# Expert 0 in two tiles of 128 rows by halves of the tokens, one of them multiplied behind the dense layers

## The chip, the cores and the metric

The kernel runs on one core of a Trainium2 chip (trn2). Time is device time in microseconds; several runs are given with their median. TensorE (PE) multiplies, VectorE (DVE) and ScalarE (ACT) work on its results, GpSimd (POOL) works in SBUF and issues the indirect DMAs, SyncE (SP) issues the other DMAs.

## The reference

Three stages, one after the other, on 1536 tokens (2 sequences of 768) of 384 features:

```python
# 1: linear attention with decay, 8 heads of 48
y[t] = r[t] @ (state + (u*k[t]) outer v[t]);  state = w*state + k[t] outer v[t]
# 2: dense layers, 384 -> 2048 -> 384
h = x @ w_in;  x2 = elu(h) @ w_out
# 3: mixture of 8 experts, one per token, capacity 384 rows each
e = argmax(x2 @ w_gate);  gate = softmax(x2 @ w_gate)[e]
out = gate * (relu(x2 @ w1[e]) @ w2[e])      # 384 -> 1024 -> 384
```

For these inputs 196 tokens choose expert 0: 96 in the first 768 tokens and 100 in the others. The fullest expert has 229.

## The kernel before, in words

Every matrix product of the dense layers and the experts is made of three fp32r products of parts (`product`, L1032): hi x hi, hi x lo, lo x hi. ScalarE makes the hi part of a weight or activation, VectorE or GpSimd the lo part.

*Dense loop.* `for n in range(NB)`: 6 blocks of 256 tokens, in each `for f in range(FT)`: 16 chunks of the 2048 features. Chunk f is 9 products of 256 columns (`fc1`, L1135) and, three chunks later, 6 products of 384 columns (`fc2`, L1149). In between go VectorE `min` (L920), ScalarE exp (L656), VectorE (L923), ScalarE g_hi (L658), GpSimd g_lo (L538). The attention of later chunks, the routing of the block before, and in block 5 the splitting of expert 0's weights (`expert0_hi` L646 for even f, `expert0_lo` L909 for odd f from 5) are placed by hand at fixed f. All engines run their lists in order; the order is written out in the code.

*Routing* of block n: `x2_rows`, `x2_transpose`, `x2_transposed`, `logits` (12 fp32 instructions of 8 columns), `shift`, `choose`, `count`, `gates`, `place_rows`, then `scatter_rows` (two indirect DMAs on GpSimd's queue) that put each token's row into the DRAM tensor `slots` at its expert's place. For blocks 0 to 4 this runs inside the next block; for block 5 nothing is left to run beside it.

*Between.* After the routing of block 5 TensorE makes `keep_busy(WARM_C)` = 9 fp32 products of 384 columns that nobody reads, waits for the scatters, makes `keep_busy(WARM_D)` = 4 more, and waits for expert 0's 256 rows. An fp32 product shows as two instructions.

*Experts.* `expert(i, r, more)` (L1264) does expert 2i+r on all engines: `expert_x` transposes its 256 rows, 8 chunks f of 9 products with 256 columns and 6 with 384. Weights of even experts lie in `we_*`, of odd ones in `wd_*`. SP loads the next weights when `fc1` (`s_he`) and `fc2` (`s_fc2e`) of the expert before last are done; at f=2 to 4 ScalarE makes the hi part of the next expert's W1 (L694), VectorE one f later the lo part (L984), at f=5 to 7 ScalarE W2 (L702), GpSimd its lo part (`split_w2`, L548). Experts with over 256 rows are finished in an overflow path that runs only if `n_over` is above 256.

## Time and profile before

| what | us |
|---|---|
| median of 3 runs | 455.81 (454.64 to 456.68) |
| profiled execution | 456.96 |
| its span | 455.2 |
| TensorE busy | 434.9 (96%) |
| VectorE busy | 243.1 (53%) |
| ScalarE busy | 183.1 (40%) |
| GpSimd busy | 235.0 (52%) |

The dense loop's last product starts at 288.2 us, expert 0's first at 307.4, expert 1's first at 325.4. Busy times of TensorE are modelled from pipelined instructions: a product's duration (0.28 us at 256 columns) is longer than the distance to the next one, so the pitch, the distance between two starts, is what a product costs. L1034, L1035 and L1036 are the three products of the helper `product`, wherever it is called from.

### The profile page before, as it was taken

The numbers are of one execution on the slowest core, as the hardware profiler recorded it, in microseconds if no ns is written. First come the engines' busy times: TensorE is split into PE (matmuls) and PEld (weight loads), VectorE is DVE, ScalarE is ACT, GpSimd is POOL, SyncE is SP. The second block draws the span as 40 slices with busy tenths as digits, with TensorE's granted clock in tenths as the row PEclk, the third lists the DMA queues.
The fourth block names the chain that finished last, engine by engine and source line by source line (L and its number), as shares of the span: only waits on it lengthen the run. The fifth ranks groups of instructions, "written<-read, shape, count | busy, mean of one in ns | idle before, by whom it ended". The sixth has DMA issues, their size and how long they took to land.

```text
span 455.2 us, 9620 instructions
## 1 busy us (share of the span) xinstructions
PE 434.9 (96%) x3796; PEld 412.9 (91%) x3796; DVE 243.1 (53%) x583; ACT 183.1 (40%) x392; POOL 235.0 (52%) x241
## 2 busy tenths in 40 slices
PE   8789999999999999999999999699999999999994
PEld 8679999999998999899999998559999999999994
DVE  7877864564465446644554575405454454553521
ACT  4255543233333333323233445104564464555520
POOL 1886785457656764675453325110725626527431
PEclk9989999999999999999999999889999999999999
DMA  7994874204111302020016002630548448357100
GB/s 255 380 403 142 291 248 177 104 8 136 37 73 25 120 16 94 18 79 2 1 29 286 0 1 56 257 104 1 208 142 329 159 186 330 114 221 291 51 30 26
DMA packets 16442, 61.80 MB, mean 136 GB/s; under 512 B 2050, under 2 KB 9118, under 8 KB 14352
## 3 DMA queue, kind: packets, MB, share of 16 engines
q1 hardware_dynamic: 14608, 56.49, 34.3%
q0 software_dynamic: 1792, 4.73, 2.8%
q8 instruction: 29, 0.48, 0.4%
q14 instruction: 13, 0.11, 0.1%
HBM read 49.38 MB, written 12.62 MB: 136 GB/s over the span
## 4 chain that ended last, share of the span: by engine, by line
PE 83%; DVE 6%; ACT 4%; DMA 2%; POOL 2%; issue 2%; SPq 0%; POOLq 0%; DVEq 0%
PE bank L1034 23%; PE bank L1036 21%; PE bank L1035 21%; PE bank L1228 2%; PE bank L1050 2%; PE bank L1075 2%; PE bank L1183 2%; ACT elu L656 1%; DMA rkt<-rkt 1%; DVE elu L923 1%; PE bank L1114 1%; PE bank L1244 1%; PE bank L1170 1%; PE bank L1110 1%; DVE we_lo L912 1%
## 5 line engine op out<-in xcount | busy, mean ns | idle before, releaser
L538 POOL TENSOR_TENSOR g_lo<-elu,g_hi 128x256 fp32r<-128x256 f32 x96 | 77.5, 807 | 106.6 <-ACT g_hi L658 106.2
L656 ACT ACTIVATE elu<-elu 128x256 f32<-128x256 f32 x96 | 40.2, 418 | 113.9 <-DVE elu L920 112.5
L1034 PE MATMUL bank<-xt,wd_hi 128*128 128x256 f32 x288 | 81.9, 284 | 1.2 <-DVE elu L923 1.2
L1035 PE MATMUL bank<-xt,wd_hi 128*128 128x256 f32 x288 | 81.4, 283 | 0.0
L1036 PE MATMUL bank<-xt,wd_lo 128*128 128x256 f32 x288 | 81.4, 283 | 0.0
L920 DVE TENSOR_SCALAR elu<-bank 128x256 f32<-128x256 f32 x96 | 40.4, 421 | 59.0 <-PE bank L1036 58.9
L1034 PE MATMUL bank<-wd_hi,g_hi 128*128 128x384 f32 x192 | 68.8, 358 | 1.5 <-POOL g_lo L538 1.5
L923 DVE SCALAR_TENSOR_TENSOR elu<-elu,bank 128x256 f32<-128x256 f32 x96 | 40.4, 421 | 49.7 <-ACT elu L656 49.7
L1035 PE MATMUL bank<-wd_lo,g_hi 128*128 128x384 f32 x192 | 64.9, 338 | 0.0
L1036 PE MATMUL bank<-wd_hi,g_lo 128*128 128x384 f32 x192 | 64.8, 337 | 0.0
L658 ACT CAST g_hi<-elu 128x256 fp32r<-128x256 f32 x96 | 39.0, 406 | 46.8 <-DVE elu L923 46.8
L977 DVE SCALAR_TENSOR_TENSOR ge_lo<-bank,ge_hi 128x256 fp32r<-128x256 f32 x64 | 27.2, 425 | 56.4 <-ACT ge_hi L689 56.4
L1034 PEld LDWEIGHTS bank<-xt,wd_hi 128*128 128x128 f32 x288 | 54.5, 189 | 2.7 <-DVE elu L923 2.3
L1036 PEld LDWEIGHTS bank<-xt,wd_lo 128*128 128x128 f32 x288 | 54.9, 191 | 0.0
L1035 PEld LDWEIGHTS bank<-xt,wd_hi 128*128 128x128 f32 x288 | 54.7, 190 | 0.0
L553 POOL TENSOR_TENSOR wd_lo<-wd_raw,wd_hi 128x1024 fp32r<-128x1024 f32 x12 | 28.5, 2403 | 46.7 <-ACT wd_hi L702 46.7
L689 ACT ACTIVATE ge_hi<-bank 128x256 fp32r<-128x256 f32 x64 | 24.7, 385 | 59.8 <-PE bank L1036 30.8
L1034 PEld LDWEIGHTS bank<-wd_hi,g_hi 128*128 128x128 f32 x192 | 36.5, 190 | 5.0 <-POOL g_lo L538 2.5
L1035 PEld LDWEIGHTS bank<-wd_lo,g_hi 128*128 128x128 f32 x192 | 36.5, 190 | 0.0
L1036 PEld LDWEIGHTS bank<-wd_hi,g_lo 128*128 128x128 f32 x192 | 36.3, 189 | 0.0
L553 POOL TENSOR_TENSOR we_lo<-we_raw,we_hi 128x1024 fp32r<-128x1024 f32 x9 | 21.4, 2402 | 24.5 <-ACT we_hi L702 24.5
L561 POOL DMA_INDIRECT out<-yrow,tok_i x16 | 15.7, 982 | 16.7 <-DVE yrow L997 13.2
(162 smaller groups left out, 978.3 us busy)
## 6 DMA issues: line engine op xcount, KB each, us to landing
we_raw<-wexp SPq DMA_DIRECT2D x8, 1536.0 KB, 7.1
wd_raw<-wexp SPq DMA_DIRECT2D x8, 1536.0 KB, 6.8
nat<-nat SPq DMA_DIRECT2D x10, 672.0 KB, 4.9
rkt<-rkt SPq DMA_DIRECT2D x12, 512.0 KB, 6.7
slots<-blank SPq DMA_DIRECT2D x2, 2316.0 KB, 11.9
xrow<-slots SPq DMA_DIRECT2D x16, 193.0 KB, 7.0
wd_raw<-win SPq DMA_DIRECT2D x4, 768.0 KB, 8.3
wd_raw<-wout SPq DMA_DIRECT2D x4, 768.0 KB, 10.4
```

What stands on the lines that cost most here:

```text
L538: nc.gpsimd.tensor_tensor(g_lo[:, f % 4, :], elu[:, f % 2, :], g_hi[:, f % 4, :].bitcast(F32), ALU.subtract).then_inc(s_glo, 1)
L553: nc.gpsimd.tensor_tensor(EL[r][:, cols], ER[r][:, cols], EH[r][:, cols].bitcast(F32), ALU.subtract).then_inc(s_elo2[r], 1)
L561: nc.gpsimd.indirect_dma_start(out=out, out_offset=bass.IndirectOffsetOnAxis(ap=tok_i[r][:, t, :], axis=0), in_=yrow[r][:, t, :], in_offse ...
L656: nc.scalar.activation(elu[:, f % 2, :], elu[:, f % 2, :], ACT.Exp).then_inc(s_exp, 1)
L658: nc.scalar.copy(g_hi[:, f % 4, :], elu[:, f % 2, :]).then_inc(s_ghi, 1)
L689: nc.scalar.activation(ge_hi[:, f % 4, :], ps_e[f % 2][:, 0:SN], ACT.Relu).then_inc(s_gehi, 1)
L920: V.tensor_scalar_min(elu[:, f % 2, :], ps_h[f % 2][:, 0:BN], 0.0).then_inc(s_m, 1)
L923: V.scalar_tensor_tensor(out=elu[:, f % 2, :], in0=elu[:, f % 2, :], scalar=-1.0, in1=ps_h[f % 2][:, 0:BN], op0=ALU.add, op1=ALU.max).then ...
L977: V.scalar_tensor_tensor(out=ge_lo[:, f % 4, :], in0=ps_e[f % 2][:, 0:SN], scalar=0.0, in1=ge_hi[:, f % 4, :].bitcast(F32), op0=ALU.max, o ...
L1034: mm(dst, w_hi, x_hi, start=start, stop=False)
L1035: mm(dst, w_hi, x_lo, start=False, stop=False)
L1036: return mm(dst, w_lo, x_hi, start=False, stop=stop)
```

## The change

Expert 0's rows are held in two tiles. Tokens of the first 768 (blocks 0 to 2, `EB` = 3) get slots 0 on, tokens of the others get slots from `LATE` = 3072 on; for that `slot0[:, 0:1]` is rewritten after block 2 from a total count (`ps_tot`), which `count` now makes for blocks 2 and 5 in front of the positions. `slots` has 27 tiles of 128 rows in place of 24.

SP loads the first tile behind expert 0's weights; TensorE transposes it at f=9 of block 5 (`early_x`), ScalarE and VectorE split it there. Behind the dense layers TensorE multiplies it (`early_fc1`, `early_fc2`: 8 chunks of 9 products with 128 columns and 3 with 384), in pieces between the routing steps of block 5 and after them. `WARM_C` goes from 9 to 2. The hi parts of expert 1's weights are made by ScalarE at early f=5 to 7 (W1) and late f=0 to 2 (W2), the lo part of W1 by VectorE in one go before the late tile. Then the second tile is loaded and multiplied in the same way as the first (late), with `expert_x` of expert 1 in it. The output rows of expert 0 are gated and scattered tile by tile. The total count for `n_over` is read on VectorE in six steps behind the early tile's gating; `n_over` is raised above 256 as well if either tile would hold over 128 rows, and the overflow path has three more turns. The diff, cut to its core:

```diff
...
-    NSB = NE * CAP // 128 // (NBLANK // 2)
+    EB = NB // 2
+    NOVER = NE + 3
+    LATE = NE * CAP
+    NSLOT = LATE + CAP
+    NSB = -(-NSLOT // 128 // (NBLANK // 2))
...
+        ps_tot = ps_y[1][:, C + 2 * BT * NE:C + 2 * BT * NE + NE]
...
-        WARM_A, WARM_B, WARM_C, WARM_D = 16, 8, 9, 4
+        WARM_A, WARM_B, WARM_C, WARM_D = 16, 8, 2, 4
...
+        F_A = 9
...
             sp.wait_ge(s_y, NSTEP)
             load_w(0, 0)
             load_w2(0, 0)
+
+            def load_part(t, row):
+                sp.dma_start(xrow[0][:, t, :], slots[row:row + 128, :]).then_inc(s_xr[0], 16)
+
+            for b in range(2):
+                sp.wait_ge(s_scat[b], 16 * BT * ((EB + 1 - b) // 2))
+            load_part(0, 0)
             sp.wait_ge(s_h, FT * NB)
             load_w(1, 1)
             load_w2(1, 1)
             for b in range(2):
                 sp.wait_ge(s_scat[b], 8 * NSTEP)
-            load_x(0, 0)
+            load_part(1, LATE)
             load_x(1, 1)
...
+                    scatter_tile(r, t)
+
+            split_w2(0, 1)
+            pool.wait_ge(s_atok, 1)
+            pool.wait_ge(s_ye[0], 1)
+            scatter_tile(0, 0)
+            pool.wait_ge(s_tok[0], 1)
+            pool.wait_ge(s_ye[0], 2)
+            scatter_tile(0, 1)
+            split_w2(1, 0)
+            scatter_out(0, 1)
+            with pool.Fori(1, NE // 2 - 1) as i:
                 split_w2(i, 1)
                 scatter_out(i, 0)
                 split_w2(i + 1, 0)
...
+                    if n == NB - 1 and f == F_A:
+                        act.wait_ge(s_axtr, 1)
+                        nc.scalar.copy(xe_hi[0][:, :, 0:C],
+                                       ps_s[0][:, 0:DM].rearrange("p (k n) -> p k n", k=KT)).then_inc(s_axhi, 1)
+
+            def early_hi(f):
+                act.wait_ge(s_ah, f + 1)
+                nc.scalar.activation(ge_hi[:, f % 4, 0:C], ps_e[f % 2][:, 0:C], ACT.Relu).then_inc(s_aghi, 1)
+
             x2_rows(NB - 1)
+            early_hi(0)
             x2_transposed(NB - 1)
+            early_hi(1)
             probs(NB - 1)
+
+
+            def expert1_hi(c):
+                act.wait_ge(s_w1[1] if c < N1 else s_w2[1], 16)
+                cols = slice(c * ECH, (c + 1) * ECH)
+                nc.scalar.copy(EH[1][:, cols], ER[1][:, cols]).then_inc(s_ehi[1], 1)
+
+            for f in range(2, ET):
+                early_hi(f)
+                if f >= ET - N1:
+                    expert1_hi(f - (ET - N1))
 
             def expert_x(i, r):
 
@@ -701,8 +764,16 @@
                         cols = slice(W1 + c * ECH, W1 + (c + 1) * ECH)
                         nc.scalar.copy(EH[nr][:, cols], ER[nr][:, cols]).then_inc(s_ehi[nr], 1)
 
-            expert_x(0, 0)
-            expert(0, 0, True)
+            act.wait_ge(s_xtr[0], 1)
+            nc.scalar.copy(xe_hi[0][:, :, C:SN],
+                           ps_xt[0][:, 0:DM].rearrange("p (k n) -> p k n", k=KT)).then_inc(s_xehi[0], 2)
+            for f in range(ET):
+                act.wait_ge(s_he, f + 1)
+                nc.scalar.activation(ge_hi[:, f % 4, 0:C], ps_e[f % 2][:, 0:C], ACT.Relu).then_inc(s_gehi, 1)
+                if f < N1:
+                    expert1_hi(N1 + f)
+                if f == F_X:
+                    expert_x(0, 1)
             expert(0, 1, True)
...
                 V.tensor_copy(slot_i[n % 2][:, :], there).then_inc(s_row, 1)
+                if n == EB - 1:
+                    link(V.tensor_copy(early0[:, :], ps_tot[:, 0:1]))
+                    link(V.tensor_scalar(slot0[:, 0:1], early0[:, :], -1.0, float(LATE), ALU.mult, ALU.add))
...
+                    if n == NB - 1 and f == F_A:
+                        dve.wait_ge(s_axhi, 1)
+                        V.tensor_tensor(xe_lo[0][:, :, 0:C], ps_s[0][:, 0:DM].rearrange("p (k n) -> p k n", k=KT),
+                                        xe_hi[0][:, :, 0:C].bitcast(F32), ALU.subtract).then_inc(s_axlo, 1)
+
+            def early_lo(f):
+                dve.wait_ge(s_aghi, f + 1)
+                V.scalar_tensor_tensor(out=ge_lo[:, f % 4, 0:C], in0=ps_e[f % 2][:, 0:C], scalar=0.0,
+                                       in1=ge_hi[:, f % 4, 0:C].bitcast(F32), op0=ALU.max,
+                                       op1=ALU.subtract).then_inc(s_aglo, 1)
+
+            def tokens_of(t, s):
+                dve.wait_ge(s_xr[0], 16 * (t + 1))
+                V.tensor_copy(tok_i[0][:, t, :], xrow[0][:, t, TOKEN:XR]).then_inc(s, 1)
+
+            def gated(t, y):
+                V.tensor_scalar(yrow[0][:, t, :], y, xrow[0][:, t, GATE:GATE + 1], None, ALU.mult).then_inc(s_ye[0], 1)
+
             x2_rows(NB - 1)
+            early_lo(0)
             x2_transposed(NB - 1)
+            early_lo(1)
             shift(NB - 1)
             choose(NB - 1)
+            early_lo(2)
             gates(NB - 1)
             place_rows(NB - 1)
-            dve.wait_ge(s_tot, 1)
-            V.tensor_reduce(col3[:, 1, 0:1], ps_y[0][:, 0:NE], AXX, ALU.max).then_inc(s_tables, 1)
-            dve.wait_ge(s_tables, NTAB + 1)
+            for f in range(3, ET):
+                early_lo(f)
+            tokens_of(0, s_atok)
+            dve.wait_ge(s_y0, 1)
+            gated(0, ps_y[0][:, 0:DM])
+            link(V.tensor_copy(part3[:, 0, :], ps_tot))
+            link(V.tensor_tensor(part3[:, 1, 0:1], part3[:, 0, 0:1], early0[:, :], ALU.subtract))
+            link(V.tensor_tensor(part3[:, 1, 1:2], part3[:, 1, 0:1], early0[:, :], ALU.max))
+            link(V.tensor_scalar_add(part3[:, 0, 0:1], part3[:, 1, 1:2], float(SN - C)))
+            link(V.tensor_reduce(col3[:, 1, 0:1], part3[:, 0, :], AXX, ALU.max))
             V.tensor_copy(n_over[:, :], col3[:, 1, 0:1]).then_inc(s_over, 1)
 
             def expert_x(i, r):
@@ -997,8 +1099,24 @@
                     V.tensor_scalar(yrow[r][:, t, :], ps_ye[t][:, 0:DM], xrow[r][:, t, GATE:GATE + 1], None,
                                     ALU.mult).then_inc(s_ye[r], 1)
 
-            expert_x(0, 0)
-            expert(0, 0, True)
+            for c in range(N1):
+                dve.wait_ge(s_ehi[1], c + 1)
+                cols = slice(c * ECH, (c + 1) * ECH)
+                V.tensor_tensor(EL[1][:, cols], ER[1][:, cols], EH[1][:, cols].bitcast(F32),
+                                ALU.subtract).then_inc(s_elo1[1], 1)
+            dve.wait_ge(s_xehi[0], 2)
+            V.tensor_tensor(xe_lo[0][:, :, C:SN], ps_xt[0][:, 0:DM].rearrange("p (k n) -> p k n", k=KT),
+                            xe_hi[0][:, :, C:SN].bitcast(F32), ALU.subtract).then_inc(s_xelo[0], 2)
+            for f in range(ET):
+                dve.wait_ge(s_gehi, f + 1)
+                V.scalar_tensor_tensor(out=ge_lo[:, f % 4, 0:C], in0=ps_e[f % 2][:, 0:C], scalar=0.0,
+                                       in1=ge_hi[:, f % 4, 0:C].bitcast(F32), op0=ALU.max,
+                                       op1=ALU.subtract).then_inc(s_gelo, 1)
+                if f == F_X:
+                    expert_x(0, 1)
+            tokens_of(1, s_tok[0])
+            dve.wait_ge(s_fc2e, ET)
+            gated(1, ps_ye[1][:, 0:DM])
...
+            def early_x():
+                pe.wait_ge(s_xr[0], 16)
+                for kt in range(KT):
+                    last = nc.tensor.transpose(ps_s[0][:, 128 * kt:128 * kt + 128],
+                                               xrow[0][:, 0, 128 * kt:128 * kt + 128], ident[:, :])
+                last.then_inc(s_axtr, 1)
+
             def x2_transpose(n, t):
                 pe.wait_ge(s_x2[t], n + 1)
                 pe.wait_ge(s_att, 2 * min(2 * n + 5, NSTEP))
+                if n == NB - 1:
+                    pe.wait_ge(s_axlo, 1)
...
                 pe.wait_ge(s_oh, n + 1)
+                if n in (EB - 1, NB - 1):
+                    pe.wait_ge(s_seen, n + 1)
+                    mm(ps_tot, ones[:, :], n_seen[:, :], start=True, stop=True)
                 mm(ps_cnt, earlier[:, :], onehot[:, :, :], start=True, stop=False)
                 mm(ps_cnt, ones[:, :], before[:, :, :], start=False, stop=True).then_inc(s_pos, 1)
...
+                    if n == NB - 1 and f == F_A:
+                        early_x()
...
+            def early_fc1(f):
+                wait_if(pe, s_aglo, f - 1)
+                if f == 0:
+                    pe.wait_ge(s_elo1[0], 2 * N1)
+                    pe.wait_ge(s_g, FT * NB)
+                for kt in range(KT):
+                    cols = slice(kt * FE + f * 128, kt * FE + (f + 1) * 128)
+                    last = product(ps_e[f % 2][:, 0:C], we_hi[:, cols], we_lo[:, cols], xe_hi[0][:, kt, 0:C],
+                                   xe_lo[0][:, kt, 0:C], kt == 0, kt == KT - 1)
+                last.then_inc(s_ah, 1)
+
+            def early_fc2(f):
+                pe.wait_ge(s_aglo, f + 1)
+                cols = slice(W1 + f * DM, W1 + (f + 1) * DM)
+                last = product(ps_y[0][:, 0:DM], ge_hi[:, f % 4, 0:C], ge_lo[:, f % 4, 0:C], we_hi[:, cols],
+                               we_lo[:, cols], f == 0, f == ET - 1)
+                if f == ET - 1:
+                    last.then_inc(s_y0, 1)
+
             for f in range(FT - LAG, FT):
                 fc2(NB - 1, f)
+            early_fc1(0)
             for t in range(BT):
                 x2_transpose(NB - 1, t)
+            early_fc1(1)
             logits(NB - 1)
+            early_fc1(2)
+            early_fc2(0)
             count(NB - 1)
-
-            pe.wait_ge(s_seen, NB)
-            mm(ps_y[0][:, 0:NE], ones[:, :], n_seen[:, :], start=True, stop=True).then_inc(s_tot, 1)
+            for f in range(3, ET):
+                early_fc1(f)
+                early_fc2(f - 2)
+            early_fc2(ET - 2)
+            early_fc2(ET - 1)
...
-            expert_x(0, 0)
-            expert(0, 0, True)
+            def late_fc2(f):
+                pe.wait_ge(s_gelo, f + 1)
+                cols = slice(W1 + f * DM, W1 + (f + 1) * DM)
+                last = product(ps_ye[1][:, 0:DM], ge_hi[:, f % 4, 0:C], ge_lo[:, f % 4, 0:C], we_hi[:, cols],
+                               we_lo[:, cols], f == 0, f == ET - 1)
+                last.then_inc(s_fc2e, 1)
+
+            pe.wait_ge(s_xr[0], 32)
+            for kt in range(KT):
+                last = nc.tensor.transpose(ps_xt[0][:, 128 * kt:128 * kt + 128], xrow[0][:, 1, 128 * kt:128 * kt + 128],
+                                           ident[:, :])
+            last.then_inc(s_xtr[0], 1)
+            pe.wait_ge(s_aglo, ET)
+            pe.wait_ge(s_xelo[0], 2)
+            for f in range(ET):
+                wait_if(pe, s_gelo, f - 1)
+                for kt in range(KT):
+                    cols = slice(kt * FE + f * 128, kt * FE + (f + 1) * 128)
+                    last = product(ps_e[f % 2][:, 0:C], we_hi[:, cols], we_lo[:, cols], xe_hi[0][:, kt, C:SN],
+                                   xe_lo[0][:, kt, C:SN], kt == 0, kt == KT - 1)
+                last.then_inc(s_he, 1)
+                if f >= 2:
+                    late_fc2(f - 2)
+                if f == F_X:
+                    expert_x(0, 1)
+            late_fc2(ET - 2)
+            late_fc2(ET - 1)
             expert(0, 1, True)
...
-            [np.concatenate([tiled(moe2_w1[e]), tiled(moe2_w2[e])], axis=1) for e in range(NE)])),
+            [np.concatenate([tiled(moe2_w1[e]), tiled(moe2_w2[e])], axis=1) for e in list(range(NE)) + [0]])),
```

## Rows read from the trace of the kernel before

**Rows 1.** Page, part 1: busy us of each engine, share of span, instructions

```profile
PE 434.9 (96%) x3796; PEld 412.9 (91%) x3796; DVE 243.1 (53%) x583; ACT 183.1 (40%) x392; POOL 235.0 (52%) x241
```

**Rows 2.** Chain of work that ended last, 262:288: start us, us, what

```profile
271.77 1.22 DVE we_lo L912
...
285.97 1.21 POOL g_lo L538
287.22 0.44 PE bank L1034
```

**Rows 3.** Timeline, 288:303: start us, us, engine, line, operation, xcount [idle before]

```profile
288.58 0.56 DVE L903 COPY x2row<-bank 128x384 f32<-128x384 f32 x1 [1.99 <-PE bank L1036]
...
289.11 0.87 PE L1170 MATMUL bank<-ident,x2row 128*128 128x128 f32 x6 [0.57 <-ACT x2row L636]
...
290.72 1.48 PE L1183 MATMUL bank<-gate_w,x2t 128*128 128x8 f32 x12 [0.74 <-DVE x2t L907]
292.31 0.17 DVE L864 TENSOR_REDUCE col<-bank 128x2 f32<-128x16 f32 x1 [1.65 <-PE bank L1183]
...
293.57 0.61 PE L1190 MATMUL bank<-onehot,earlier 128*128 128x16 f32 x2 [1.37 <-DVE before L873]
...
295.59 0.17 DVE L898 CAST slot_i<-prob 128x2 uint32<-128x2 f32 x1
...
301.44 1.75 SPq L388 DMA_DIRECT2D xrow<-slots  x4
```

**Rows 4.** Chain of work that ended last, 280:330, the idling products

```profile
295.02 10.96 PE bank L1228 x26
```

**Rows 5.** Source view of L388, 300:307: the first four row loads

```profile
DMA to landing us min/median/max: 2.5/2.9/3.7
```

**Rows 6.** Timeline, 306:311.5: first product of expert 0 and three later ones

```profile
307.41 0.36 PE L1278 MATMUL bank<-xe_hi,we_hi 128*128 128x256 f32 x1 [0.77 <-ACT xe_hi L681]
...
310.97 0.28 PE L1036 MATMUL bank<-xe_hi,we_lo 128*128 128x256 f32 x1
...
311.09 0.34 PE L1034 MATMUL bank<-we_hi,ge_hi 128*128 128x384 f32 x1
...
311.27 0.34 PE L1035 MATMUL bank<-we_lo,ge_hi 128*128 128x384 f32 x1
```

**Rows 7.** Timeline, 322:330: weight load, first product of expert 1, first use

```profile
322.66 0.35 SPq L381 DMA_DIRECT2D we_raw<-wexp  x1
...
325.44 0.28 PE L1278 MATMUL bank<-xe_hi,wd_hi 128*128 128x256 f32 x1
...
329.24 1.04 ACT L694 CAST we_hi<-we_raw 128x1024 fp32r<-128x1024 f32 x1
```

**Rows 8.** Groups by line and form, weight loads: xcount, busy us, mean ns

```profile
L1035 PEld LDWEIGHTS bank<-xe_lo,we_hi 128*128 128x128 f32 x84 | 15.8, 188 | 0.0
...
L1075 PEld LDWEIGHTS bank<-nat 128*64 128x64 f32 x320 | 10.2, 138 | 3.4 <-POOL nat L467 1.6 <-issue 0.9
L1183 PEld LDWEIGHTS bank<-gate_w,x2t 128*128 128x128 f32 x72 | 8.5, 191 | 1.6 <-issue 1.5
```

**Rows 9.** Groups by line and form, VectorE

```profile
L984 DVE TENSOR_TENSOR wd_lo<-wd_raw,wd_hi 128x1024 fp32r<-128x1024 f32 x12 | 14.6, 1216 | 0.0
...
L814 DVE TENSOR_TENSOR xt<-bank,xt 128x128 fp32r<-128x128 f32 x12 | 3.4, 281 | 0.0
...
L907 DVE COPY x2t<-bank 128x384 f32<-128x384 f32 x6 | 3.3, 552 | 0.9 <-PE bank L1170 0.9
```

**Rows 10.** Groups by line and form, ScalarE

```profile
L640 ACT COPY x2t<-bank 128x384 f32<-128x384 f32 x6 | 2.8, 473 | 0.6 <-PE bank L1170 0.6
```

**Rows 11.** Timeline, 28:31.5, TensorE

```profile
28.42 1.12 PE L1075 MATMUL bank<-nat 128*64 128x32 f32 x32 [1.36 <-POOL nat L467]
```

**Rows 12.** Windows: stretch, us, TensorE busy, granted clock, DMA share, GB/s

```profile
30.00:33.40 3.40, 3.40 (x16) 0.53 1.02 413
...
294.00:300.00 6.00, 6.00 (x13) 0.51 0.18 66
```

More of the change, by code:

```diff
@@ L89, in build @@
     col3 = new("col3", [128, 2, BT])
+    early0 = new("early0", [128, 1])
     slot_i = [new(f"slot_i{b}", [128, BT], U32) for b in range(2)]
@@ L108, in build, with expert_rows @@
     end_d = top[0]
+    def expert_rows(r):
+        return (new(f"xrow{r}", [128, 2, XR]), new(f"xe_hi{r}", [128, KT, SN], F32R),
+                new(f"xe_lo{r}", [128, KT, SN], F32R), new(f"yrow{r}", [128, 2, DM]),
+                new(f"tok_i{r}", [128, 2, 1], U32))
+    rows0 = expert_rows(0)
+    end_d = top[0]
     top[0] = x_at
-    xrow = [new(f"xrow{r}", [128, 2, XR]) for r in range(2)]
-    xe_hi = [new(f"xe_hi{r}", [128, KT, SN], F32R) for r in range(2)]
-    xe_lo = [new(f"xe_lo{r}", [128, KT, SN], F32R) for r in range(2)]
     ge_hi = new("ge_hi", [128, 4, SN], F32R)
     ge_lo = new("ge_lo", [128, 4, SN], F32R)
-    yrow = [new(f"yrow{r}", [128, 2, DM]) for r in range(2)]
-    tok_i = [new(f"tok_i{r}", [128, 2, 1], U32) for r in range(2)]
+    xrow, xe_hi, xe_lo, yrow, tok_i = zip(rows0, expert_rows(1))
     assert max(top[0], end_d) <= nc.sbuf_usable_end, (top[0], end_d)
@@ L238, in build @@
         s_sout = pair("out_scattered")
+        s_axtr = sem("early_x_transposed")
+        s_axhi = sem("early_x_hi_ready")
+        s_axlo = sem("early_x_lo_ready")
+        s_ah = sem("early_h_done")
+        s_aghi = sem("early_g_hi_ready")
+        s_aglo = sem("early_g_lo_ready")
+        s_atok = sem("early_tok_ready")
         s_dld = sem("d_loaded")
@@ L414, in _, with load_over @@
             with sp.If(over > SN):
-                def load_over(e):
+                def load_over(e, row):
                     sp.dma_start(we_raw[:, :], wexp[bass.ds(e, 1), :, :]).then_inc(s_dld, 16)
-                    sp.dma_start(xrow[0][:, 0, :], slots[bass.ds(e * CAP + SN, 128), :]).then_inc(s_dld, 16)
-                load_over(0)
-                with sp.Fori(1, NE) as e:
+                    sp.dma_start(xrow[0][:, 0, :], slots[bass.ds(row, 128), :]).then_inc(s_dld, 16)
+                load_over(0, SN)
+                with sp.Fori(1, NE + 1) as e:
                     sp.wait_ge(s_dout, 16 * e)
-                    load_over(e)
-                sp.wait_ge(s_dout, 16 * NE)
+                    load_over(e, e * CAP + SN)
+                with sp.Fori(0, 2) as j:
+                    sp.wait_ge(s_dout, 16 * (j + NE + 1))
+                    load_over(j * NE, j * LATE + C)
+                sp.wait_ge(s_dout, 16 * NOVER)
         @block.gpsimd
@@ L516, in scatter_rows @@
                 pool.wait_ge(s_row, n + 1)
-                pool.reg_add(last_slot, one, NE * CAP - 2)
+                pool.reg_add(last_slot, one, NSLOT - 2)
                 nc.gpsimd.indirect_dma_start(
@@ L554, in split_w2, with scatter_tile @@
                                             ALU.subtract).then_inc(s_elo2[r], 1)
+            def scatter_tile(r, t):
+                pool.reg_add(last_token, one, T - 2)
+                nc.gpsimd.indirect_dma_start(
+                    out=out, out_offset=bass.IndirectOffsetOnAxis(ap=tok_i[r][:, t, :], axis=0),
+                    in_=yrow[r][:, t, :], in_offset=None, bounds_check=last_token,
+                    oob_is_err=False).then_inc(s_sout[r], 16)
             def scatter_out(i, r):
@@ L559, in scatter_out @@
                     pool.wait_ge(s_ye[r], 2 * i + t + 1)
-                    pool.reg_add(last_token, one, T - 2)
-                    nc.gpsimd.indirect_dma_start(
-                        out=out, out_offset=bass.IndirectOffsetOnAxis(ap=tok_i[r][:, t, :], axis=0),
-                        in_=yrow[r][:, t, :], in_offset=None, bounds_check=last_token,
-                        oob_is_err=False).then_inc(s_sout[r], 16)
-            with pool.Fori(0, NE // 2 - 1) as i:
+                    scatter_tile(r, t)
[9 more added lines that the diff above has]
+            with pool.Fori(1, NE // 2 - 1) as i:
                 split_w2(i, 1)
@@ L576, in _ @@
             with pool.If(over > SN):
-                with pool.Fori(0, NE) as e:
+                with pool.Fori(0, NOVER) as e:
                     pool.wait_ge(s_dye, e + 1)
@@ L714, in _ @@
             with act.If(over > SN):
-                with act.Fori(0, NE) as e:
+                with act.Fori(0, NOVER) as e:
                     act.wait_ge(s_dld, 32 * (e + 1))
@@ L1010, in _ @@
             with dve.If(over > SN):
-                with dve.Fori(0, NE) as e:
+                with dve.Fori(0, NOVER) as e:
                     dve.wait_ge(s_dhi, e + 1)
@@ L1305, in _ @@
             with pe.If(over > SN):
-                with pe.Fori(0, NE) as e:
+                with pe.Fori(0, NOVER) as e:
                     pe.wait_ge(s_dld, 32 * (e + 1))
```

11 lines of the change are left out of this document (6 added, 5 removed).

## The prediction

> **What bounds the kernel now.** I read the page's busy shares first: TensorE is busy 434.9 of 455.2 us [rows 1], so what can still be won lies where it works on nothing useful. The chain of work that ended last says where that is. It runs on TensorE through nearly the whole span; the exceptions are the last dense block and the stretch behind it. In the second half of the last dense block the chain goes through VectorE: at f=9 the placing of rows and a 1.22 us split of expert 0's weights hold back the next `elu` step, and the chain stays on VectorE, ScalarE and GpSimd until 287.2, where the last dense products start [rows 2]. Six of these at the pitch of 0.175 us end at D = 288.4.
>
> Then the timeline from D to the first product of expert 1 at 325.44 [rows 3, 6, 7]. Routing the last block takes TensorE some 2.6 us of work in 6 us of waiting; the slots are known at 295.76; the two scatters land and the row loads start at 301.44 [rows 3]; the rows land 2.5 to 3.7 us later [rows 5]; expert 0 starts at 307.41 [rows 6] and lasts 18.0 us. From 295.02 to 305.98 TensorE only idles with 13 products that nobody reads (26 instructions) [rows 4], over half of it at half clock [rows 12]. So 325.44 − 288.4 = 37.1 us, of which 19 carry no expert work. Half an expert fits in there. From expert 1 on, TensorE is the bound again and nothing of the order changes, so the shift of expert 1's start is the change in time.
>
> **The pitch of a product.** The halves multiply 128 columns of rows where the old form multiplied 256. In fp32r, products of 256 columns follow each other every 0.12 us (0.118 over long runs), those of 384 every 0.175 [rows 6]. No row shows one of 128. If columns alone counted, the line through the two gives 0.061. But each product loads its own 128 weight columns: the fp32r load lasts 188 ns, the fp32 load 191 with 128 columns and 138 with 64 [rows 8], so 64 columns cost 53 ns and 128 columns 107. And 12 products of only 8 columns take 1.48 us, with 0.25 for the last one by itself (a little under the 0.28 of 256 columns [rows 6]) a pitch of (1.48−0.25)/11 = 0.112 [rows 3]: that is the load, as the product has next to no columns. So below 256 columns I take a flat 0.113, the row that shows the load by itself. The other end is the plain fp32 rate: the idling products, two instructions each, run at some 0.33 us an instruction of 384 columns at full clock, by columns 0.11 at 128 and 0.22 for a product in two [rows 4]. The bounds are 0.061 and 0.22.
>
> **Part by part.** (1) *Dense layers.* Fetching the early rows adds three transposes to TensorE (0.34 us), a copy to ScalarE (0.47, as L640) [rows 10] and a subtraction of 384 columns to VectorE (0.55, as L907) [rows 9], all at f=9 of the last block. VectorE there is on the chain [rows 2], so its 0.55 counts in full; the transposes hide in TensorE's waits that this chain makes, and ScalarE is idle there. The total count of block 2 is two more small fp32 instructions in block 3, 0.23 us, where TensorE is the bound. The load of the early rows is queued on SP behind expert 0's weights, long after blocks 0 to 2 were scattered, and some 25 us ahead of its use; it holds back nothing. The two new small VectorE steps in block 3 and three more blank blocks cost 0 (the blanks are due at the first scatter, tens of us later); without that cover 0.4. Sum +0.8, bounds 0.2 and 1.5.
>
> (2) *From D to the early result.* TensorE's list: 72 products at 0.113 = 8.1; 24 at 0.175 = 4.2; six transposes, twelve logit and six counting instructions at 0.113 = 2.7; and 0.3 for the new wait on the running count, behind which the counting and all later products queue. Sum 15.3. The routing chain is pushed back by the interleaved pieces: 0.3 at the transposes, then 0.1 at the logits (fc1(1) is in front), 0.5 as VectorE must do early_lo(2) (0.28, as L814 [rows 9]) before the gates and waits for fc1(2). The slots are known some 0.7 later; loads start at 302.1 and land by 305.8, before they are needed. The round trip of a chunk (0.27 product, 0.3 ScalarE, 0.28 VectorE, gaps) is 0.9 us and has 1.6 to 2.1, also with a 1.04 us weight copy [rows 7] between.
>
> (3) *Between the halves.* The idling falls from 13 products to 6: 12 instructions at 0.33 = 4.0; with transposes (0.35+0.16), ScalarE (0.5), VectorE (0.6) and the gaps TensorE could start the late half 5.9 after the early result. But VectorE has a longer queue from there: 0.2 to start, gating 0.56, six small links at 0.2 = 1.2, three splits of expert 1's weights that were hidden in expert 0 before, 3 x 1.22 = 3.7 [rows 9], xe_lo 0.55, 0.15 to TensorE: 6.4. That sets the start. Here the stall goes to: VectorE is late next, not the rows.
>
> (4) *Late half.* 8.1 + 4.2 + 0.7 of transposes for expert 1 = 13.0, against 18.0 for the whole expert. Expert 1's W2 copies (ScalarE, f=0 to 2) and GpSimd's splits start earlier relative to their use than before.
>
> Sum: 15.3 + 6.4 + 13.0 = 34.7 against 37.1, −2.4; with +0.8, −1.6. One more thing moves: expert 2's W1 load was issued 2.8 us before expert 1 starts and used 3.8 after it [rows 7]; now the last fc1 is nearer the end and it is issued 1.4 before. ScalarE may wait 1 to 1.7 us for it; its result is due 2 us later, so I count 0, at most 0.5.
>
> The profiled execution took 456.96 (455.2 span, 1.8 around it), 1.15 over the median of 455.81. It would become 455.4; on the median −1.6 gives **454.2**.
>
> On the pitch the Trainium skill says otherwise. "TensorE: Matmul & The Clock Gate", section "Back-to-back issue gap", gives about 81 ns for a sustained stream of loads and products with 128 columns. By that the sum would be 144 x 0.032 = 4.6 us lower; the 8-column row here, 0.112, speaks against it, though that one is fp32.
>
> **Rivals.**
> *A. Narrow products are cheaper than the load row says.* At 0.08, 144 x 0.033 = 4.8 us less: 449.4. At 0.061 the arrival of the late rows takes over: the late half can't start before 305.8+0.8+1.7 = 308.3 instead of 310.9, and saves another 3.7 itself: 454.2−2.6−3.7 = 447.9. For: the products' own columns. Against: rows 8 and the 8-column row.
> *B. Narrow fp32r products run at the fp32 rate.* At 0.22, 144 x 0.107 = 15.4 more: **469.6**, clearly slower. The point from which the change loses is a pitch of 0.113 + 1.6/144 = 0.124. For: no row of the kernel has an fp32r product under 256 columns, and its fp32 ones are all in two slow instructions. Against: the loads of fp32r and fp32 last alike, so one load explains 0.113.
> *C. The clock falls.* TensorE stands 2 us before the late half. In the trace an idle stretch of 1.36 us before light work [rows 11] was followed by 3.2 us at half clock [rows 12]; a fall here costs half of that, 1.6: 455.8. If it falls in the routing stage as before (half clock for 6 us of 294 to 300 [rows 12]), half of 6 us, 3.0: 457.2. Against the latter: the stretch has two full groups of products in its gaps now.
> *D. It doesn't do what it says.* If over 128 tokens of a half choose expert 0, the overflow path runs eleven turns, at least 100 us. The reference's routing for these inputs gives 96 and 100, so no. Or a wait that I don't see makes the early half run behind the routing, up to +3: 457.
>
> **How the numbers follow.** Forecast 454.2, its own range 452.7 to 455.7 from the bounds of parts 1 to 4: chance 0.48. C 0.22, A 0.09, B 0.12, D and the rest 0.09. About 0.5% (2.3 us: 453.5 and 458.1) is what a measurement of this kernel can tell from no change. Faster: a third of the forecast's case, all of A: 0.24. Slower: B and small tails of C and D: 0.18. Within: 0.58. The range of 8 in 10 takes the forecast, C and D and leaves out B and most of A: 451.5 to 458.0.
>
> **What the profile will show.** Right: fc1 groups of 128 columns at 0.11 to 0.12; early result near 304.5; a 2 us gap of TensorE before the late half with VectorE's `wd_lo` splits in it; expert 1 at about 323.9; slots known at about 297.3; last dense product 0.6 to 0.8 later. Wrong: another pitch; a granted clock of 0.5 anywhere from 288 to 325; the late half released by the row load.

## The result

| | before | after |
|---|---|---|
| median of the runs, us | 456.25 (454.64 to 458.36, 4 runs) | 470.9 (468.8 to 473.14, 4 runs) |
| profiled execution: time / span, us | 456.96 / 455.2 | 471.28 / 469.6 |
| D, the end of the last dense products | 288.4 | 289.86 |
| slots known | 295.76 | 298.23 |
| first row load of the last rows | 301.44 | 303.08 |
| first product of expert 1 | 325.44 | 339.47 |

The changed kernel takes 1.032 times as long (95% interval 1.0254 to 1.0384): 14.7 us slower, where 1.6 faster was forecast. Several kernels below, the changed one too, have fast and slow runs according to whether, and for how long, TensorE's clock falls in expert 0; where the two mix the single times are given.

The page of after, TensorE's busy time and, in 40 slices of 11.7 us, the tenths of full clock that were granted:

```profile
PE 451.0 (96%) x3856; PEld 431.5 (92%) x3856; DVE 244.2 (52%) x598; ACT 183.8 (39%) x400; POOL 234.9 (50%) x241
PEclk9789999999999999999999999557699999999998
```

Against [rows 1] TensorE is busy 16.1 us longer with 60 instructions more; VectorE, ScalarE and GpSimd did not change by more than 1.1. More busy time without more work means slower work, and the clock row says where: two slices of 5, one of 7 and one of 6, between 293 and 340. The windows of TensorE cut that stretch at the moments where the clock changes (columns: stretch, us, busy us and instructions, granted clock as a share of 2.4 GHz, DMA share, GB/s):

```profile
289.86:294.70 4.84, 4.84 (x46) 1.00 0.60 256
294.70:313.00 18.30, 18.30 (x77) 0.50 0.17 55
313.00:322.00 9.00, 7.62 (x34) 0.87 0.00 0
322.00:335.00 13.00, 13.00 (x58) 0.51 0.03 12
335.00:343.00 8.00, 8.00 (x60) 0.95 0.41 135
```

In the first row the new early half runs at full clock. Then 18.3 us of it run at 1.2 GHz. The clock is back during the idling products between the halves, which are dense and 384 columns wide, and falls again for 13 us of the late half. It comes back while the late half's products of 128 columns still run, 3.7 us before expert 1 begins:

```profile
335.52 0.41 PE L1152 MATMUL bank<-xe_hi,we_hi 128*128 128x128 f32 x1
335.73 0.32 PE L1153 MATMUL bank<-xe_lo,we_hi 128*128 128x128 f32 x1
335.89 0.27 PE L1154 MATMUL bank<-xe_hi,we_lo 128*128 128x128 f32 x1
```

Half of 18.3 + 13.0 is 15.7, about the size of the whole loss.

The timeline of after, at the stations of the prediction's sum:

```profile
289.85 0.22 PE L1152 MATMUL bank<-xe_hi,we_hi 128*128 128x128 f32 x1
...
298.06 0.17 DVE L969 CAST slot_i<-prob 128x2 uint32<-128x2 f32 x1
...
303.08 0.33 SPq L415 DMA_DIRECT2D xrow<-slots  x1
...
313.38 5.00 PE L1385 MATMUL bank<-x2t,ones 128*128 128x384 f32 x12
...
315.19 3.49 DVE L1105 TENSOR_TENSOR wd_lo<-wd_raw,wd_hi 128x1024 fp32r<-128x1024 f32 x3
...
318.22 0.49 PE L1461 MATMUL bank<-ident,xrow 128*128 128x128 f32 x3
...
319.38 0.56 DVE L1108 TENSOR_TENSOR xe_lo<-bank,xe_hi 128x384 fp32r<-128x384 f32 x1 [0.71 <-ACT xe_hi L768]
...
339.47 0.28 PE L1435 MATMUL bank<-xe_hi,wd_hi 128*128 128x256 f32 x1
```

The early half ends where the idling begins, at 313.38: 23.5 us after D. Between the halves it is 6.7 to 320.1, and the late half takes 19.4 to 339.47. Together 49.6 us from D to expert 1, where the kernel before has 37.1 and the forecast 34.7. The arrival of the last rows, issued at 303.08, decides nothing any more.

### The profile page after: what moved, and what is told of

It is laid out like the page before. It is cut to its first block, busy times and chain, and to the rows that moved or that the text cites. A ratio compares the mean times of both kernels' runs of the same rounds, so it can differ in the third digit from the quotient of the medians.

```text
span 469.6 us, 9759 instructions
## 1 busy us (share of the span) xinstructions
PE 451.0 (96%) x3856; PEld 431.5 (92%) x3856; DVE 244.2 (52%) x598; ACT 183.8 (39%) x400; POOL 234.9 (50%) x241
## 4 chain that ended last, share of the span: by engine, by line
PE 81%; DVE 6%; DMA 4%; ACT 3%; POOL 2%; issue 2%; SPq 1%; POOLq 0%; DVEq 0%; ACTq 0%
PE bank L1152 23%; PE bank L1154 22%; PE bank L1153 21%; PE bank L1193 2%; PE bank L1168 2%; DMA xrow<-slots 2%; PE bank L1310 2%; ACT elu L697 1%; DMA rkt<-rkt 1%; DVE elu L997 1%; PE bank L1401 1%; PE bank L1228 1%; PE bank L1232 1%; PE bank L1297 1%; DVE we_lo L986 1%
## 5 line engine op out<-in xcount | busy, mean ns | idle before, releaser
L1079 DVE SCALAR_TENSOR_TENSOR ge_lo<-bank,ge_hi 128x256 fp32r<-128x256 f32 x56 | 23.8, 425 | 50.2 <-ACT ge_hi L752 50.2
L752 ACT ACTIVATE ge_hi<-bank 128x256 fp32r<-128x256 f32 x56 | 21.5, 385 | 49.1 <-PE bank L1154 28.8
L1152 PE MATMUL bank<-xe_hi,we_hi 128*128 128x256 f32 (+1 forms) x111 | 34.7, 313 | 1.4 <-DVE xe_lo L1108 1.4
```

What stands on the lines that cost most here:

```text
L752: nc.scalar.activation(ge_hi[:, f % 4, :], ps_e[f % 2][:, 0:SN], ACT.Relu).then_inc(s_gehi, 1)
L1079: V.scalar_tensor_tensor(out=ge_lo[:, f % 4, :], in0=ps_e[f % 2][:, 0:SN], scalar=0.0, in1=ge_hi[:, f % 4, :].bitcast(F32), op0=ALU.max, o ...
L1152: mm(dst, w_hi, x_hi, start=start, stop=False)
```

## The experiments

Two explanations stood against each other. *The clock*: the narrow products cost what they should (0.11 us), but a stream of them does not bring TensorE back from 1.2 GHz, so a fall lasts as long as the half. *The queues*: a wait (VectorE's queue between the halves, the new wait on the running count) holds the halves up and the clock only follows. The trick that tells them apart: stream each half's 128 columns of rows twice, so that a fc1 product has 256 columns. By the load-bound pitch that costs nothing, the columns streamed a second time land in the unused half of the bank, and all waits and queues stay as they are.

**Both halves wide (wide_both).**

```diff
-last = product(ps_e[f % 2][:, 0:C], we_hi[:, cols], we_lo[:, cols], xe_hi[0][:, kt, 0:C],
-               xe_lo[0][:, kt, 0:C], kt == 0, kt == KT - 1)
+last = product(ps_e[f % 2][:, 0:SN].rearrange("p (a n) -> p a n", a=2), we_hi[:, cols], we_lo[:, cols],
+               xe_hi[0][:, kt, 0:C].unsqueeze(1).to_broadcast([128, 2, C]),
+               xe_lo[0][:, kt, 0:C].unsqueeze(1).to_broadcast([128, 2, C]), kt == 0, kt == KT - 1)
```

The helpers of the edit are written out here. The late half has the same edit with C:SN.

> The changed kernel with each of the 144 narrow fc1 products of expert 0 streaming its 128 columns twice (256 columns, the second half of the result is not used); nothing else differs. Theory T (a stream of 128-column products, each as long as its weight load, leaves TensorE's clock at 1.2 GHz): the granted clock stays near 1.0 from 289 to 340, pitch 0.118, and the time falls from 470.9 to about 455.5. Rival R (the clock falls by the light routing work behind the dense layers and by the pause ahead of the late half, whatever the width): clock 0.5 as before, time 469 to 472. Rival B (a narrow fp32r product is itself slow): would also give about 455, but the trace of the changed kernel has shown 0.11 us at full clock for it, so the clock's part would be no more than 1 us.

Measured: 455.06 (452.85 to 455.7, 10 runs) beside 455.95 of before; ratio 0.9977 (0.9951 to 1.0003). The loss is gone, 15.8 us by the medians, with no wait touched. Its windows from D to expert 1, all engines (busy us of PE, PEld, DVE, ACT, POOL, then clock, DMA share, GB/s):

```profile
288.00:303.50 15.50, 15.50 (x121) 15.23 (x121) 6.41 (x31) 6.20 (x14) 1.96 (x2) 1.00 0.35 131
303.50:309.40 5.90, 4.39 (x18) 2.55 (x16) 5.35 (x11) 0.48 (x1) 0.00 (x0) 1.00 0.13 46
309.40:322.70 13.30, 13.30 (x102) 13.27 (x103) 3.32 (x11) 5.69 (x13) 8.10 (x4) 1.00 0.03 12
```

At a clock of 1.00 throughout, the three stages take 15.5, 5.9 and 13.3 us. The forecast had 15.3, 6.4 and 13.0: the same sum of 34.7, in part because misses of 0.2 to 0.5 cancel. Between the halves the timeline shows which engine is late:

```profile
303.51 4.03 PE L1391 MATMUL bank<-x2t,ones 128*128 128x384 f32 x12
...
305.29 3.48 DVE L1105 TENSOR_TENSOR wd_lo<-wd_raw,wd_hi 128x1024 fp32r<-128x1024 f32 x3
...
308.69 0.55 DVE L1108 TENSOR_TENSOR xe_lo<-bank,xe_hi 128x384 fp32r<-128x384 f32 x1
...
309.38 0.36 PE L1152 MATMUL bank<-xe_hi,we_hi 128*128 128x256 f32 x1 [1.51 <-DVE xe_lo L1108]
```

VectorE leaves its three splits at 308.7 and goes straight into `xe_lo`; ScalarE's `xe_hi` had been there for some 0.2 us. So VectorE's queue does set the start, but by 0.2 us, not by the 0.5 that was forecast; the 5.9 us are what the forecast had for TensorE's own path.

**One half wide at a time (wide_early, wide_late).** The same edit in the early or in the late half alone.

> Only the 72 fc1 products of the early half stream 256 columns. T: the early result comes 8 us sooner, the late half stays at half clock: 470.9 - 8 = 462 to 463. R: 469 to 472.

> Only the 72 fc1 products of the late half stream 256 columns. T: the late half takes 13.5 us in place of 19.4, the early half stays at half clock: 470.9 - 6 = 464 to 465. R: 469 to 472.

Measured, early half wide: 455.48 (454.56 to 463.01, 10 runs), ratio 0.9998 (0.9976 to 1.002) without the slowest; nine of the ten lie between 454.6 and 457.2 and one at 463.0. The 462 to 463 that was expected came once in ten. Late half wide: 462.7, 465.48, 465.2 and 453.92. The windows of the latter, all engines:

```profile
288.80:294.90 6.10, 6.10 (x52) 5.78 (x51) 3.42 (x15) 2.01 (x6) 0.00 (x0) 0.95 0.50 212
294.90:311.90 17.00, 17.00 (x72) 17.00 (x73) 2.91 (x16) 4.19 (x8) 1.96 (x2) 0.51 0.19 59
...
317.70:331.10 13.40, 13.35 (x102) 13.35 (x103) 3.32 (x11) 5.69 (x13) 8.11 (x4) 1.00 0.04 12
```

With a narrow early half the clock falls at about 294.3, as in after at 294.8, and stays down for 17 us; the wide late half then runs at 1.00 in 13.4. So a narrow early half loses by itself, 8 to 10 us over wide_both in three runs of four. A narrow late half behind a wide early half seldom loses. Why is not shown: in after too the clock was up when the late half began, and fell 2 us later.

**Which part of the early half (wide_first3, wide_last5).** Chunks 0 to 2 lie between the pieces of routing, chunks 3 to 7 behind them.

In short:

```diff
+if f < 3:      # wide_first3: these wide, all else narrow
+if f >= 3:     # wide_last5: these and the late half wide
```

> Of the changed kernel's 144 narrow products only the 27 of early chunks 0 to 2, which stand between the routing steps of the last block, stream 256 columns; the other 117 stay at 128. Theory T2 (the clock falls in the light stretch of the routing, some 294 us, and narrow products only fail to bring it back): the clock stays up, 455 to 456. Theory T1 (a stream of narrow products lowers the clock by itself): it falls a few us later, 462 to 470.

> The reverse: early chunks 0 to 2 stay at 128 columns, early chunks 3 to 7 and the whole late half stream 256. T2: the clock falls near 294.7 as in the changed kernel, and the wide products behind it bring it back in some 5 us, as the idling products did in the kernel before: 2.5 us lost, about 457.5. T1 (only the stream matters): it hardly falls, 455 to 456. If a fallen clock stays down whatever follows until a pause: 463 to 465.

Measured, the first three wide: 453.23, 453.32, 454.86, 455.01, 455.1, 455.19, 459.28, 463.9, 464.05, 464.37 and 465.38. All but the first three wide: 455.32 (454.57 to 457.62, 10 runs), ratio 0.9977 (0.9949 to 1.0006). The profiled execution of wide_first3 is the slowest of its eleven; TensorE's windows:

```profile
289.00:304.50 15.50, 15.50 (x124) 1.00 0.35 130
304.50:310.40 5.90, 4.39 (x17) 1.00 0.18 61
310.40:333.60 23.20, 23.20 (x102) 0.53 0.07 18
```

The narrow chunks 3 to 7 run at full clock here, and the early half takes 15.5 us as in wide_both. After the middle stretch, in which TensorE stands 1.5 us, the clock falls and the narrow late half takes 23.2 us instead of 13.3. With the same three chunks narrow and everything behind them wide, no run is over 457.62, and the profiled one has 1.00 throughout; a fall and a quick return, the expected 457.5, fits at most its two slowest runs (457.3 and 457.62). So it is not one place of the kernel: a fall costs much where a narrow stretch follows it; whether the clock falls differs from run to run.

**Does a narrow stream lower the clock by itself (steady_narrow)?** The kernel before, with expert 1's fc1 as twice as many products of 128 columns, in the middle of dense work:

```diff
+for t in range(2):
+    half = slice(t * 128, (t + 1) * 128)
+    for kt in range(KT):
+        last = product(ps_e[f % 2][:, half], EH[r][:, tile[kt]], EL[r][:, tile[kt]],
+                       xe_hi[r][:, kt, half], xe_lo[r][:, kt, half], kt == 0, kt == KT - 1)
```

> The kernel before, with one edit: the 72 fc1 products of expert 1, in the middle of the dense stream of expert products, are made as 144 products of 128 columns, one half of the rows after the other. No light work, no pause beside them. Theory T1 (a stream of narrow products lowers the clock by itself): granted clock 0.5 through expert 1, its 17.7 us become some 46, the time 480 or more. Theory T2 (a fall needs light work or a pause first; narrow products then fail to bring the clock back): clock 1.0, and only the doubled number costs, 144 x 0.113 - 72 x 0.118 = 7.8: 464.5.

Measured: 463.81 (463.49 to 465.46, 4 runs), ratio 1.0156 (1.0105 to 1.0208). TensorE's windows over expert 0, the narrowed expert 1 and expert 2, and two of its narrow products:

```profile
306.96:325.00 18.04, 18.02 (x126) 1.00 0.10 29
325.00:350.50 25.50, 25.50 (x203) 1.00 0.43 160
350.50:368.00 17.50, 17.50 (x127) 1.00 0.57 215
```

```profile
330.31 0.28 PE L1034 MATMUL bank<-xe_hi,wd_hi 128*128 128x128 f32 x1
330.42 0.27 PE L1035 MATMUL bank<-xe_lo,wd_hi 128*128 128x128 f32 x1
```

25 us of narrow work at a clock of 1.00: here the stream alone doesn't lower a clock that stands high. And its pitch is 0.11. By the timeline expert 1 takes 25.1 us (325.00 to 350.08) and expert 2 17.7, so that 72 more products cost 7.4 us (7.0 by the medians): a 128-column product is nearly as dear as one of 256. In a narrow form the work of two halves costs twice, which the forecast had in its 144 products.

**Does a narrow stream raise a fallen clock (routing_first_narrow, routing_first_wide)?** The early chunks 0 to 2 are put behind the routing on every engine, so that TensorE has the light routing stretch of the kernel before ahead of the early half, where that kernel's clock fell. The halves are then narrow or wide.

```diff
-early_fc1(0)
 for t in range(BT):
     x2_transpose(NB - 1, t)
-early_fc1(1)
 logits(NB - 1)
-early_fc1(2)
-early_fc2(0)
 count(NB - 1)
+early_fc1(0)
+early_fc1(1)
+early_fc1(2)
+early_fc2(0)
```

> The changed kernel with the early chunks 0 to 2 moved behind the routing steps of the last block on all engines, so that the routing runs alone, as in the kernel before, and the early half is one stream of 128-column products behind it. In the kernel before the clock falls in that stretch in every profile (near 293) and the idling products bring it back in some 6 us. T2 (narrow products do not bring it back): granted clock 0.5 from about 5 us behind the dense layers to the idling products, the early half at half pitch throughout: 25 us for it, the time 470 to 478. If narrow products bring the clock back as well: some 3 us lost over routing_first_wide at most, 458 to 462.

> The same with both halves at 256 columns. T2: the clock falls at the same place and the wide products bring it back in 3 to 6 us: the early result comes 22 us behind the dense layers (6.3 routing, 12.7 products, 3 lost to the clock) and not 15.5: 455.1 + 6.5 = 461.5. If wide products don't bring it back: as the narrow one, over 468.

Measured: narrow 471.0 (467.16, 467.93, 474.08 and 474.38), ratio 1.03 (1.0199 to 1.0401); wide 461.64 (459.82 to 464.58, 10 runs), ratio 1.0093 (1.0056 to 1.013). TensorE's windows, narrow:

```profile
286.00:293.50 7.50, 4.53 (x30) 0.90 0.50 211
293.50:316.35 22.85, 22.85 (x98) 0.51 0.14 44
316.35:322.00 5.65, 4.36 (x16) 1.00 0.00 0
322.00:335.00 13.00, 12.78 (x101) 1.00 0.04 13
```

and wide:

```profile
287.00:295.00 8.00, 5.03 (x30) 0.75 0.48 203
295.00:298.00 3.00, 3.00 (x15) 0.52 0.00 0
298.00:309.00 11.00, 11.00 (x84) 1.00 0.28 91
```

Both start the early half with the clock down. With products of 256 columns it is back after 3 us. With products of 128, which run without a gap (22.85 of 22.85 us busy), it stays down for 22 us and is back at 315.9, in the nine products of 384 columns that end the half, just ahead of the idling at 316.35. This is the mechanism of the loss, shown on both sides. It is no rule without exception: in the late half of after, and of after_again below, the clock came back 13.6 us behind the fall, among products of 128 columns. What differs there is not shown.

**VectorE's order (wide_order).** The forecast held that VectorE's three splits of expert 1's weights delay the late half. Here they are moved behind the first `ge_lo` steps of the late half.

```diff
-for c in range(N1):            # ahead of the late xe_lo
-    expert1_lo(c)
 V.tensor_tensor(xe_lo[0]...)
 for f in range(ET):            # late half
     ge_lo(f)
+    if f < N1:
+        expert1_lo(f)
```

> Both halves at 256 columns, and on VectorE the lo part of the late rows goes ahead of the three splits of expert 1's W1, which follow late chunks 0 to 2. If VectorE's queue sets the start of the late half once the clock is up (step 3 of the prediction), TensorE's pause shrinks by 0.5 to 0.7 us and the time is that much under wide_both, about 454.9. If not, it is the same as wide_both.

Measured: 458.57 (456.15 to 460.67, 10 runs), ratio 1.0057 (1.0026 to 1.0089), so 3.5 us worse than wide_both and not 0.5 better. From the timeline:

```profile
311.63 1.22 DVE L1105 TENSOR_TENSOR wd_lo<-wd_raw,wd_hi 128x1024 fp32r<-128x1024 f32 x1
...
312.41 6.04 POOL L582 TENSOR_TENSOR wd_lo<-wd_raw,wd_hi 128x1024 fp32r<-128x1024 f32 x2 [12.93 <-ACT wd_hi L734]
...
312.96 3.24 DVE L1105 TENSOR_TENSOR wd_lo<-wd_raw,wd_hi 128x1024 fp32r<-128x1024 f32 x1
...
316.46 0.39 PE L1155 MATMUL bank<-xe_hi,we_hi 128*128 128x256 f32 x1 [1.19 <-DVE ge_lo L1113]
```

The same split takes 1.22 us alone and 3.24 beside GpSimd's split; the `ge_lo` behind it comes late and TensorE stands 1.19 us, and 1.48 at the next one. The saving at the start was 0.1 us (5.74 from the idling to the late half in place of 5.87), and the late half takes 16.6 us in place of 13.3. The Trainium skill has this as a rule: "SBUF — State Buffer", section "SBUF: two separate sides", says that a VectorE operation with two inputs in SBUF and a GpSimd operation that reads SBUF exclude each other for the length of an instruction. The 1.22 and 3.24 are in keeping with it.

**The splits where VectorE is free (wide_vec_c0d1, wide_vec_fa).** They go into the early half instead, where GpSimd has next to no work (1.96 of 15.5 us in wide_both's first window); the steps that count overflowing rows go behind the late gates; and the idling between the halves is cut from 6 products to 1, since a wide stream needs none. In wide_vec_fa the early `xe_lo` also moves from f=9 to f=10, off VectorE's chain of [rows 2].

```diff
 for f in range(ET):            # early half
     ge_lo(f)
+    if f == ET - 2:
+        expert1_lo(0)
+expert1_lo(1)
+expert1_lo(2)
-WARM_C, WARM_D = 2, 4
+WARM_C, WARM_D = 0, 1
-if n == NB - 1 and f == F_A:       # wide_vec_fa only
+if n == NB - 1 and f == F_A + 1:
```

> Both halves at 256 columns; VectorE splits expert 1's W1 among the early chunks 6 and 7, while GpSimd rests, and counts for n_over behind the late half; the idling products between the halves go from 6 to 1. The late half then starts 2.4 us behind the early result and not 5.9: 455.1 - 3.5 = 451.6. Rival: the rows of the second tile land later than that, and the gain is 2 or less (453); or the shorter run-up lets the clock fall, 453 to 457.

> As wide_vec_c0d1, and the subtraction for the early rows on VectorE goes from f=9 to f=10 of the last dense block, where VectorE waits 1.4 us for ScalarE. If its 0.5 us is on the chain as the prediction has it, 0.5 less: 451.1; if not, the same as wide_vec_c0d1.

Measured: wide_vec_c0d1 451.62 (450.18 to 453.41, 5 runs), ratio 0.9898 (0.9866 to 0.9931); wide_vec_fa 450.85 (449.73 to 453.65, 5 runs), ratio 0.9871 (0.984 to 0.9902). The two can't be told apart, so whether the early `xe_lo` was on the chain stays open here; the second has the lowest median here, 1.3% under before. The timeline of the first, between the halves:

```profile
301.58 2.35 DVE L1059 TENSOR_TENSOR wd_lo<-wd_raw,wd_hi 128x1024 fp32r<-128x1024 f32 x2
...
302.43 0.81 PE L1399 MATMUL bank<-x2t,ones 128*128 128x384 f32 x2
...
304.43 0.55 DVE L1115 TENSOR_TENSOR xe_lo<-bank,xe_hi 128x384 fp32r<-128x384 f32 x1
...
305.13 0.36 PE L1160 MATMUL bank<-xe_hi,we_hi 128*128 128x256 f32 x1 [1.57 <-DVE xe_lo L1115]
```

The late half starts 2.7 us after the early result instead of 5.9; 3.2 us less, which is the gain over wide_both (3.4 by the medians, each on its own chip). The data had been there all along: of the 5.9 us, most was idling work and VectorE's queue.

**The same order with narrow halves (narrow_vec_c0d1), and the changed kernel again (after_again).** With less time between the halves, does the narrow form lose less?

> The changed kernel's 128-column products as they were, with VectorE's new order and one idling product between the halves. If the clock falls in the early half as in the changed kernel, the 4 us between the halves are saved and the rest stays: 466 to 468. Where it holds: 451 to 452. A time under 460 in most runs would say that the idling products had a part in the falls.

> The changed kernel once more, on the chip of the two others, for how often its clock falls. T2: as before, 468 to 473 in nearly all runs, at times 463 (one half spared) or 455 (both). T1: 468 to 473 always.

Measured, narrow with the new order: 451.07, 451.77, 453.17, 454.04, 456.41, 457.49, 458.44, 458.67, 464.3 and 468.02. The changed kernel: 455.25, 467.72, 469.4 and 469.9. The fast ends are those of a clock that did not fall (mean granted clock 0.993 in the run of 451.07, 0.989 in that of 455.25, against 0.948 in the profiled run of after). So the changed kernel reaches the forecast, 454.2, within 1.1 us in one of its eight runs, and lies 13.5 to 18.9 us above it in the others.

Eight of the ten runs with the new order lie under 460. By what was written ahead of the run that would say that the idling products had a part in the falls. The runs don't show it: on TensorE the kernel is the same as after until the idling, and after's first fall, at 294.8, lies ahead of all that was changed. Nor is the spread from 453 to 459 explained; falls shorter than those of the traces would fit it, but only the run of 451.07 was traced.

## Why the prediction was wrong

**The pitch: right.** A flat 0.113 was taken from the row of 8-column products in [rows 3]. In after, at full clock and then at half:

```profile
291.55 0.28 PE L1153 MATMUL bank<-xe_lo,we_hi 128*128 128x128 f32 x1
291.66 0.27 PE L1154 MATMUL bank<-xe_hi,we_lo 128*128 128x128 f32 x1
...
297.17 0.41 PE L1153 MATMUL bank<-xe_lo,we_hi 128*128 128x128 f32 x1
297.38 0.42 PE L1154 MATMUL bank<-xe_hi,we_lo 128*128 128x128 f32 x1
```

0.11 at 2.4 GHz and 0.21 at 1.2. Rival A (0.06 to 0.08) and rival B (0.22) both fall. B's time, 469.6, is near the measured 470.9, but for another reason: the 0.21 that would seem to prove it stands only in the stretches of clock 0.5, and the first 4.84 us of the same half have 0.11. The nearness is chance; whoever had looked at the time alone would have called B right.

**Part 1, dense layers, +0.8: right in kind, a little high.** The chain of after goes through the new subtraction, behind the split of `we_lo`, as was forecast:

```profile
272.78 1.22 DVE we_lo L986
274.00 0.47 DVE xe_lo L1031
274.46 0.34 DVE elu L994
```

That is the 0.5 of it. D came 1.5 later than in before; 1.0 of that was there ahead of the subtraction already (272.78 for 271.77 in [rows 2]), and wide_both, with the same dense layers, has D at 288.0, earlier than before's 288.4. So execution by execution D moves by as much as this term, and its other 0.23 can't be read.

**Part 2, D to the early result, 15.3: right at full clock, 23.5 in after.** wide_both has 15.5, wide_first3 too. The 8.2 more are the 18.3 us at half clock. TensorE has no gap there, so the new wait on the running count cost nothing that shows.

**Part 3, between the halves, 6.4 set by VectorE: 5.9, and VectorE ahead by only 0.2.** The links and splits took what was forecast; VectorE had begun some of them earlier, beside the idling. In after it is 6.7, as the twelve idling instructions, partly at half clock, take 5.00 instead of 4.03, and VectorE waits 0.71 for `xe_hi`: there TensorE sets the start.

**Part 4, late half, 13.0: 13.3 at full clock, 19.4 in after.** The difference is again the clock.

**The clock was the step that failed.** The sum priced every product at full clock: the clock stood in it at nothing, and at 1.6 to 3.0 us only in rival C. The fall was named there, its place was right (the routing stage at 294, and the stretch behind TensorE's stand before the late half), and it had a chance of 0.22. Its size was wrong: it came from the 3.2 and 6 us at half clock of [rows 12]. The halves run at half clock for 18.3 and 13 us here, at a cost of 8.2 + 0.3 + 6.4 = 14.9 of the 15.9 us between the profiled execution and its forecast of 455.4, and most runs have such falls. The error lay in carrying the length of a fall over from before. In the kernel before, what follows a fall in the routing stage is the 26 dense idling instructions of 384 columns [rows 4], and the clock is back 5 us into them, at little cost, as nobody reads these products; the change takes these away from there and puts the narrow products of the expert in their place. The argument against C, that the stretch "has two full groups of products in its gaps now", did not hold: TensorE was busy without a gap for the 4.84 us before the fall. The chance was too low for what came, seven runs of eight. A granted clock of 0.5 between 288 and 325 was a sign of being wrong that the forecast had named. The range ended at 458.0 since it had only this size of C, and left B out.

**Part by part at full clock** the forecast stands: 34.7 from D to expert 1 in the forecast and in wide_both; wide_both's median lies 0.9 under before where 1.6 was forecast, and its ratio's interval, 0.9951 to 1.0003, doesn't exclude no gain at all.

What stays open: what makes the clock fall in one run and not in the next. In after TensorE stood 1.29 us at 287.4, 7 us ahead of the fall; wide_both stands the same 1.29 us there and doesn't fall; wide_last5, which has the same narrow chunks 0 to 2 as wide_late, shows no long fall in ten runs, though a short one would not show in its times. In the thirty runs of the kernels with both halves wide and after's order of routing (wide_both, wide_order, wide_vec_c0d1, wide_vec_fa) no mean granted clock is under 0.985, against 0.945 to 0.962 in seven of the changed kernel's eight: wide products have no long fall in any run, but short ones can't be excluded. The runs settle what a fall costs, not what starts it.

## What to carry to other kernels

When a change makes TensorE's products narrower, price a fall of its clock by what stands behind it, not by how long falls lasted before: here narrow, load-bound products kept a high clock up for 25 us and left a low one down for 13 to 22. If such products must follow a light stretch or a pause, stream the columns twice up to the width at which the load is hidden: here going from 128 to 256 columns cost next to nothing and gave 15 us back. And before cutting idling work, ask which products bring the clock back in its place.

## What the runs showed of the hardware

- Products in fp32r with a new load of 128 x 128 weights each have a pitch of 0.11 us with 128 columns of rows and 0.12 with 256; 72 more of them in steady_narrow cost 7.4 us. On this the Trainium skill, "TensorE: Matmul & The Clock Gate", section "Back-to-back issue gap", has about 81 ns for 128 columns; in a stream of them no run here shows less than 0.11.
- At a granted clock of 0.5 the narrow pitch is 0.21, twice that at 1.00 (after).
- A fallen clock was back within 3 us of 256-column products (routing_first_wide). Under chunks of nine 128-column and three 384-column products, with TensorE busy without a gap, it stayed down for 17 us in wide_late and 22 in routing_first_narrow, to the nine 384-column products at the end of the half, and for 22 us, to the end of the late half, in wide_first3; in the late halves of after and after_again it came back after 13.6. The same chunks left a clock of 1.00 alone for 25 us (steady_narrow).
- A VectorE split of 128 x 1024 takes 1.22 us alone and 3.2 beside a GpSimd split (wide_order).
